# The first megabyte of the second expert's weights moved from SyncE's queue to ScalarE's, inside the first turn of the expert loop

## What is computed

```python
attn_out = _attn_ref(**attn_kwargs)
x = np.ascontiguousarray(attn_out.transpose(0, 2, 1, 3)).reshape(B * S, H * D)
...
h = np.maximum(np.einsum('ecd,edf->ecf', disp, w1), 0.0)
y = np.einsum('ecf,efd->ecd', h, w2)
...
out[i] = gate_w[i] * y[expert_idx[i], pos[i]]
...
h = x @ w_in
sp = np.where(h > 20.0, h, np.log1p(np.exp(np.minimum(h, 20.0))))
g = h * np.tanh(sp)
return (g @ w_out).astype(np.float32)
```

## Time and profile before

| what | value |
|---|---|
| median of 3 runs | 412.69 us (412.6 to 412.78) |
| profiled execution, its own time | 412.77 us |
| its span | 411.0 us |
| PE busy | 397.0 us (97% of the span) |
| DVE, ACT, POOL busy | 249.9, 200.3, 81.4 us |
| moved by DMA | 62.85 MB, mean 153 GB/s |

### The profile page before, as it was taken

The page is one execution under the profiler, slowest core; times in us unless marked ns, Lnnn a source line. Parts: engine busy times, 40 slices in busy tenths (PEclk is TensorE's granted clock), DMA queues, the critical chain, the costliest instruction groups (busy, mean ns, idle before and its releaser), DMA issues.

```text
span 411.0 us, 7244 instructions
## 1 busy us (share of the span) xinstructions
PE 397.0 (97%) x2666; PEld 365.1 (89%) x2668; DVE 249.9 (61%) x442; ACT 200.3 (49%) x388; POOL 81.4 (20%) x81
## 2 busy tenths in 40 slices
PE   8899999999999899899999999999999999999995
PEld 3688898898999789799999999999988999899984
DVE  5888989989989541201101111118899998877761
ACT  5968968968778220210110110117667555553441
POOL 1910320320600050474534600000000000000005
PEclk9999999999999999999999999999999999999999
DMA  8856913972600055999899999900000000000003
GB/s 299 268 119 186 233 21 81 306 164 66 218 2 0 8 203 176 425 410 337 306 349 348 362 347 382 332 9 0 2 0 0 2 2 2 0 0 2 0 2 153
DMA packets 15451, 62.85 MB, mean 153 GB/s; under 512 B 2112, under 2 KB 2752, under 8 KB 11328
## 3 DMA queue, kind: packets, MB, share of 16 engines
q1 hardware_dynamic: 14032, 58.51, 42.2%
q0 software_dynamic: 960, 3.15, 2.0%
q10 hardware_dynamic: 432, 0.83, 0.5%
HBM read 49.89 MB, written 3.15 MB: 129 GB/s over the span
## 4 chain that ended last, share of the span: by engine, by line
PE 51%; DMA 4%; DVE 4%; ACT 2%; issue 1%; POOL 1%; POOLq 0%; SPq 0%; DVEq 0%
PE ps L814 14%; PE ps L714 13%; PE ps L730 12%; PE ps L789 12%; DMA ring<-in_w 2%; DMA rows<-xg,sloti 1%; DVE nt__120 L1310 1%; ACT lt L1024 1%; DVE nt__120 L1293 1%; ACT at__119 L1027 1%; DVE hn L1315 1%; DVE hn L1308 1%; ACT et L1012 0%; POOL rows L457 0%; DVE at__119 L1290 0%
## 5 line engine op out<-in xcount | busy, mean ns | idle before, releaser
L714 PE MATMUL ps<-xs,ring 128*128 x512 | 60.0, 278 | 1.6 <-DMA ring<-in_w 1.2
L714 PEld LDWEIGHTS ps<-xs,ring 128*128 128x128 f32 x512 | 58.5, 191 | 3.0 <-issue 3.0
L730 PE MATMUL ps<-hs,ring 128*128 128x128 f32 (+1 forms) x512 | 59.2, 276 | 0.0
L730 PEld LDWEIGHTS ps<-hs,ring 128*128 128x128 f32 x512 | 58.5, 192 | 0.0
L1172 DVE TENSOR_TENSOR ptl<-ps,pth 128x384 fp32r<-128x384 f32 x96 | 48.8, 550 | 4.3 <-ACT pth L937 4.2
L937 ACT ACTIVATE pth<-ps 128x384 fp32r<-128x384 f32 x96 | 42.2, 495 | 18.6 <-PE ps L648 18.0
L1115 DVE TENSOR_REDUCE nmax<-ps 128x1 f32<-128x768 f32 x48 | 45.7, 955 | 4.2 <-PE ps L534 2.6
L534 PE MATMUL ps<-ops 128*128 128x384 f32 x192 | 44.4, 352 | 1.4 <-ACT prob L899 1.4
L899 ACT ACTIVATE prob<-ps,nmax 128x768 f32<-128x768 f32 x48 | 43.5, 907 | 1.7 <-DVE nmax L1115 1.6
L789 PE MATMUL ps<-yh,wih 128*128 128x384 f32 x128 | 43.1, 336 | 0.3 <-ACT hc L1016 0.3
L648 PE MATMUL ps<-cfs,prob 128*128 128x128 f32 x288 | 41.3, 276 | 1.8 <-DVE ptl L1172 1.5
(11 more groups left out here) (160 smaller groups left out, 677.5 us busy)
## 6 DMA issues: line engine op xcount, KB each, us to landing
ring<-in_w SPq DMA_DIRECT2D x32, 1024.0 KB, 7.7
winraw<-in_w_in SPq DMA_DIRECT2D x8, 512.0 KB, 7.6
woutraw<-in_w_out SPq DMA_DIRECT2D x8, 512.0 KB, 8.7
ops<-kh SPq DMA_DIRECT2D x12, 192.0 KB, 3.4
ops<-qh SPq DMA_DIRECT2D x6, 384.0 KB, 5.7
xg<-rows SPq DMA_DIRECT2D x1, 1539.0 KB, 7.2
raw<-in_vt SPq DMA_DIRECT2D x4, 384.0 KB, 5.1
raw<-in_qt SPq DMA_DIRECT2D x3, 384.0 KB, 6.7
```

The lines of the kernel that those rows point to most:

```text
L714: last = mm(ps[:, fc // 2, (fc % 2) * WIDE:(fc % 2) * WIDE + W], wa[:, 2 * fc // KF, kd, P * (fc % (KF // 2)):P * (fc % (KF // 2)) + P], x ...
L730: last = mm(ps[:, 4 + half * KD // 2 + k, 0:W], wb[:, half, fc, P * k:P * k + P], hs[:, fc, 0:W], start=(fc == 0), stop=(fc == KF - 1))
```

## The change

It adds a semaphore, lets ACT issue half 0 of the second expert's `wa` in turn 0, between its two `hs` copies, once `Hw` has reached 2, and makes SP leave out that transfer in its first turn. The bytes, the buffer and the semaphore that PE waits for (`wa0`) stay the same, and so does every later turn apart from a branch in ACT's and in SP's loop.

```diff
+        def first_half_weights(engine, e, half):
+            engine.dma_start(wa[:, half, :, :], w1[bass.ds(e, 1), half, :, :, :].rearrange(
+                "o p c n -> (o p) c n")).then_inc(s[f"wa{half}"], 16)
...
             def first_weights(e, half):
-                sp.dma_start(wa[:, half, :, :], w1[bass.ds(e, 1), half, :, :, :].rearrange(
-                    "o p c n -> (o p) c n")).then_inc(s[f"wa{half}"], 16)
+                first_half_weights(sp, e, half)
...
             with sp.Fori(0, E - 1) as i:
-                for half in range(2):
-                    hold(sp, s["passed_sp"], s["Hw"], 4 * i + 2 * half + 2)
-                    first_weights(i + 1, half)
+                with sp.If(i > 0):
+                    hold(sp, s["passed_sp"], s["Hw"], 4 * i + 2)
+                    first_weights(i + 1, 0)
+                hold(sp, s["passed_sp"], s["Hw"], 4 * i + 4)
+                first_weights(i + 1, 1)
...
                         av(hs[:, 2 * b:2 * b + 2, 0:W],
                            ps[:, b, 0:2 * WIDE].rearrange("p (a c) -> p a c", a=2)[:, :, 0:W],
                            ACT.Relu).then_inc(s["Ha"], 1)
+                        if b == 0:
+                            with act.If(e < 1):
+                                hold(act, s["passed_act"], s["Hw"], 2)
+                                first_half_weights(act, 1, 0)
```

More of the change, by code:

```diff
@@ L216, in attention_moe_mish @@
         sems = {}
-        for n in ["first_" + n for n in MISH_A + MISH_B] + ["still", "c0", "c", "cr", "k0", "q0", "k1", "q1", "pj", "pj2", "passed_sp", "passed_gp", "rk0", "rk1", "rv0", "rv1", "ca", "cq", "cp", "pja", "pjb", "ah", "ab", "ao", "ak", "aq", "ka", "kl", "ks", "ch", "cc", "opsA", "opsB", "wa0", "wa1", "wb0", "wb1", "Yc", "wi", "wo", "out",
+        for n in ["first_" + n for n in MISH_A + MISH_B] + ["still", "c0", "c", "cr", "k0", "q0", "k1", "q1", "pj", "pj2", "passed_sp", "passed_act", "passed_gp", "rk0", "rk1", "rv0", "rv1", "ca", "cq", "cp", "pja", "pjb", "ah", "ab", "ao", "ak", "aq", "ka", "kl", "ks", "ch", "cc", "opsA", "opsB", "wa0", "wa1", "wb0", "wb1", "Yc", "wi", "wo", "out",
                   "pjh", "pjl", "wg",
```

## The result

The changed kernel takes 414.4 us (median of 20 runs, 413.06 to 416.94), the kernel before 412.65 us in the same comparison (20 runs, 411.76 to 413.44): ratio 1.0044, 95% interval 1.0031 to 1.0057. The forecast was 412.2 us, slightly faster, with a range up to 413.5. The change costs 1.75 us.

What follows compares the result with a forecast made beforehand. PE was taken to bound the kernel, busy 97% of the span at full clock. A gain of 0.79 us less a scatter delay of 0.31 made −0.48 us, so 412.2 us, range 411.8 to 413.5.

Steps and rivals of the forecast that it cites:

- The load wait goes whole: Start of the second turn: the earlier transfer lands between 159.8 and 167.3, before PE wants it at 168.62.
- Gain: 0.79 us: Start of the second turn: the fourth matmul begins at 169.51 instead of 170.295, then limited by DVE's last `xs` copy.
- ACT issues at about 154.65: Turn 0, after ACT's first `hs` and `Hw` = 2: issue 4.75 us sooner than SP's at 159.40.
- The scatter in flight: DMA engines near 155.6: the megabyte meets the last scatter and delays its landing, by 0.31 us in the forecast.
- d: Delay of the last scatter's landing, added in full to the total: 0.31 us, bounds 0 and 2.5.
- rival B: DMA engines at 155.6: three to eight megabyte packets precede the scatter's end, delay 0.8 to 2.5, 412.8 to 414.4; chance 0.19.
- if it takes other than its 7.2 us: Sign that the forecast is wrong: a read-back time different from 7.2 us; no cost was given for it.
- rival C: Change fails: ACT issues late, or the transfer's end meets the read-back; nothing gained if landing after 169.4, 412.7; chance 0.06.
- ACT's issue, the branch, SP: 0: ACT's issue and later branch fit its 3.19 us idle gap; SP's changed queue keeps nobody on PE waiting: cost 0.

Runs made afterwards that it cites:

- quarter: Changed kernel with only 256 KB of the megabyte issued early on ACT's queue, 768 KB by SP behind the read-back: 411.64 us against 411.63 before, ratio 0.9991.
- base: The kernel before, unedited, profiled again on chip C: 411.46 us in one execution, its 28 runs between 410.82 and 413.16.
- pool: Against the kernel before: megabyte fetched near 132 us into a spare tile, copied into place by POOL, no early ACT issue; chip B, 411.15 us, ratio 0.9992.
- base2: The kernel before, unedited, profiled a third time, on chip D: 412.17 us in the profiled execution, 412.12 over its runs.
- again4: The changed kernel, unedited, on chip D: 414.23 us against 412.12 for the kernel before, ratio 1.0058.
- again3: The changed kernel, unedited, on chip C: 412.21 us against 411.63 for the kernel before, ratio 1.0015.
- sbuf: Changed kernel with the early megabyte read from a tile of zeros in SBUF instead of DRAM; chip B, 413.54 us, ratio 1.006 to the kernel before.
- half: Changed kernel with half the megabyte issued early, the rest by SP behind the read-back; chip B, 412.89 us, ratio 1.0043 to the kernel before.
- again: The changed kernel, unedited, on chip A: 413.68 us against 411.92 for the kernel before, ratio 1.0054.
- tiny: Changed kernel with the early transfer cut to 64 KB, so stale weights are used; chip A, 411.57 us, ratio 0.9994 to the kernel before.
- spearly: Megabyte issued early by SP, ahead of its wait for the scatters, with ACT's loop as before; chip A, 414.34 us, ratio 1.0055 to the kernel before.
- again5: The changed kernel, unedited, on chip E: 414.39 us against 412.13 for the kernel before, ratio 1.0049.
- warm: Changed kernel plus eight matmuls of zeros ahead of PE's wait for the read-back; chip C, 412.8 us against 411.63 for the kernel before, ratio 1.0029.
- warm2: Changed kernel plus eight matmuls of zeros ahead of PE's wait for the read-back, on chip E: 413.87 us, ratio 1.0044 to the kernel before.
- late: Changed kernel with ACT issuing the megabyte only once the scatters have landed; chip B, 415.38 us against 411.48 before, ratio 1.0115.
- code: Changed kernel keeping branches and waits but without the early issue; SP issues half 0 in its old place; chip A, 412.18 us, ratio 1.0002 to before.
- pool2: Kernel with the megabyte fetched near 132 us and copied by POOL, run on chip D: 411.32 us against 412.12 for the kernel before, ratio 0.9982.

## Why the prediction was wrong, by its own steps

**"The load wait goes whole": right, but it was no constant.** It is gone in every profile with the early issue but quarter's, where the 768 KB left behind kept 0.6 us of it. But the forecast took 1.25 us of idle time from one profile for a property of the kernel. base has none of it. In such an execution the change has nothing to win. That fits pool, which removes the wait, delays neither transfer and gains only 0.3 and 0.8 us on its two chips.

**"Gain: 0.79 us": mis-sized where the wait exists.** It was 0.98 us in the first pair and, from base2 (176.70 − 168.14 = 8.56) and again4 (177.88 − 170.21 = 7.67), 0.89 on chip D. The last slice of `xs` was taken for the fourth record of L714. The "64 matmuls in eight groups of four" of the part ahead are 64 records of 32 matmuls, two for each; the slice is needed at the seventh record, where the chain after breaks ("x6", then "x58"). With 172.72 − 172.58 (the end of the last `xs` copy, 171.89 + 0.69) = 0.14 us behind the copy, and 170.54 (177.28 − 6.74) before, the sum would have given 0.99. That DVE's `xs` is late next was right.

**"ACT issues at about 154.65": right on chip C, wrong in the profile of record.** ACT and DVE began their first `hs` 1.3 to 3.2 us later on four of the five chips and in the changed kernel's own profile. Nothing in the first profile of before could show this. The issue then falls at 156.1 to 156.6.

**"The scatter in flight": the sign was right, the size depends on the chip.** Where the issue came at 154.7 to 155.0, as planned, d was 0.8 us (again3) and, with a quarter of the bytes, 1.3 us (quarter) against base, not 0.31: rival B's range. Each rests on one profile, and the first profile of before, with no early issue, had 4.63 us itself. The place of the collision was wrong as well: in again3 no packet of the megabyte moved before 156.5, 1.5 us after its issue, and from then to 157 none of the scatter's. Where the issue came late, d was 0.6 on chip A, −0.1 on chip D, 0 on chip B (sbuf, half). The reading behind the 0.31, that the landing waits for a packet of code, is not borne out: in base2 such a packet starts between 157.2 and 157.3 us and takes 0.912 × 1.6 = 1.46 us, and the scatter landed at 158.02, before its end.

```profile
q8 instruction: 1, 0.02, 91.2%
```

**The failed step is the read-back.** The forecast wrote "if it takes other than its 7.2 us" among the things that would prove it wrong, and gave it no price. It looked for a collision with the transfer ahead; the one with the read-back stands only in half a sentence of rival C, where it costs no more than the gain (412.7) and has a share of 0.06. By the forecast's figures a megabyte of 2.5 us, on the engines from 155.6, is through at 158.1; but even in again3, issued on time, 19 of its packets moved from 159 to 159.5. It was issued 2 us late and began at over 1.1 us for a packet instead of 0.31, so it still held the DMA engines when the read-back came. The read-back took 1.6 us more in the first pair, 1.5 on chip A (again against tiny), 2.0 on chip D, and only 0.3 on chip C (again3 against base), where the issue came on time. Rival B named the right resource and a wrong victim: the same mechanism, with the read-back in the place of the scatter. Its prices (412.8 to 414.4) hold the result, but that is luck: with its own victim, the scatter, late by 0.96 us it gives 412.9. It had 0.19.

The read-back loses this time at two places. In again4 it starts late (no packet for 2.4 us). In the first pair most of it is lost at the end. Packets in the microsecond before its last one, in the profile before (164.36 to 165.36) and in the changed kernel's (167.55 to 168.55):

```profile
DMA packets 192, 0.47 MB, mean 468 GB/s; under 512 B 15, under 2 KB 15, under 8 KB 175
DMA packets 58, 0.40 MB, mean 401 GB/s; under 512 B 0, under 2 KB 0, under 8 KB 12
```

Before, 175 − 15 = 160 packets of the read-back move in it, ten for each of 16 engines; after, 12, one engine's work, while the others are at the next load. By the records of the single packets 752 of the 768 were through 0.6 us later after the issue than before, the last one 1.66 us later. And a packet of code lies inside the changed kernel's read-back, from 161 to 162 us, where before it had come at 156.5, ahead of it:

```profile
q8 instruction: 1, 0.02, 6.0%
```

It takes 0.96 us of one engine. It is so in all four profiles with a read-back of 8.8 us or more behind a full megabyte issued before the scatter landed and read from DRAM (changed, spearly, again4, again5); in again, again3, warm and warm2 it comes before 160 us, and they have 8.7, 7.5, 7.4 and 7.9. Again shows that the megabyte costs 1.5 us without it. How much of the first pair's 1.6 us belongs to the packet of code, and whether the megabyte pushed it there, was not tested.

**The clock had no place in the forecast.** In the two profiles in which PE's new wait was 3.6 us (spearly, again5) the clock fell to 1.2 GHz and the transposes took 1.7 us more. In the two with 3.0 us (the changed kernel's first profile, late) it stayed at 2.4 GHz.

**"ACT's issue, the branch, SP: 0": right.** code shows it for the branches, tiny for the issue. The cover that the prediction named, `Hw` late by less than 1.2 us, was gone on the chips with late signals: in again4 ACT's `hs` of bank 2 starts 5.96 us after PE's first matmul (156.61 − 150.65), in base2 5.66. PE's wait for the read-back hides it.

In sum: +1.0 (scatter) + 1.6 (read-back) − 0.98 (load wait) = +1.6 us for the first pair of profiles, against −0.48 forecast, plus 0.4 that lies outside the change's steps (the later start of 0.58 us, partly given back). What decides is that the megabyte was moved from behind the read-back, where it delayed nothing before the second turn, to just ahead of it. A version that beats both kernels beyond doubt was not found: pool's intervals both reach 1.

## What to carry to other kernels

A transfer on another queue is not out of the way of the critical one: it shares the 16 DMA engines. A megabyte already on them held up the first packet of the critical transfer (again4); issued together, as in late, the two mixed and the critical one was later still. A transfer ends with its last engine, so a packet of code on one of the 16 can cost a microsecond. Before a prefetch is moved ahead of a wait, work out when its last byte is through in the worst case and which critical transfer is issued by then; if they meet, move it to a stretch in which the DMA engines idle, even at the price of a copy. A wait of about a microsecond in a single profile is worth a second profile before it is taken for the gain.

## What the runs showed of the hardware that was not expected

- ACT began its first `hs` 2.1 us after PE's first matmul of the loop on one chip, 3.7 on another and 5.2 to 5.3 on three others, with PE busy throughout; the changed kernel itself showed 2.1, 3.7 and 5.2.
- The first 8 KB packets of a transfer from DRAM took over 1.1 us each, behind the scatter (again4, sixteen packets, 1.18 us) and after 10 us of idle DMA engines (pool2, eight packets, 1.13 us); from SBUF 0.33 us (sbuf).
- A scatter of 128 rows landed 3.4 to 5.6 us after its issue, by chip and by what followed it.
- A packet of code takes 1.0 to 1.5 us of one DMA engine (0.96 us and 1.46 us in base2). In three of the four profiles with the load in its old place the load's last small packet came over a microsecond behind the others, and PE waited 1.1 to 1.2 us; that a packet of code is the cause is read from the rows of base and base2, not tested.
- PE's clock fell to half once PE went on after a wait of 3.6 us (spearly, again5), not after 3.0 us (the changed kernel's first profile, late), and stayed there until about 173 us, some 3 us.
